# Attention and two mixture layers on one core: the values of dilated pairs are loaded from GpSimd's queue

## The reference

```python
scores = scale * np.matmul(q, k.transpose(0, 1, 3, 2))
rel = pos[:, None] - pos[None, :]
mask_plain = (rel >= 0) & (rel < 32)
mask_dil = (rel >= 0) & (rel < 128) & (rel % 4 == 0)
# heads 0..3 use mask_plain, heads 4..7 mask_dil
attn = softmax(scores under the mask); x = (attn @ v) as rows of 512
# layer 1: each row goes to one of 8 experts (by its cosine to expert_emb), relu(x @ w1[e]) @ w2[e], times a gate
# layer 2: h = x @ w_in; out = (h * cos(h)) @ w_out
```

## Time and profile before

| | us |
|---|---|
| median of 3 runs | 856.87 |
| lowest and highest | 856.0, 858.98 |
| the profiled execution | 854.68 |
| span of its trace | 852.8 |
| TensorE busy | 823.2 (97%) |
| VectorE busy | 608.7 (71%) |
| ScalarE busy | 489.9 (57%) |
| GpSimd busy | 75.7 (9%) |

### The profile page before, as it was taken

The page is one execution under the profiler, slowest core; times in us unless marked ns, Lnnn a source line. Parts: engine busy times, 40 slices in busy tenths (PEclk is TensorE's granted clock), DMA queues, the critical chain, the costliest instruction groups (busy, mean ns, idle before and its releaser), DMA issues.

```text
span 852.8 us, 15550 instructions
## 1 busy us (share of the span) xinstructions
PE 823.2 (97%) x5046; PEld 753.6 (88%) x5046; DVE 608.7 (71%) x1187; ACT 489.9 (57%) x948; POOL 75.7 (9%) x129
## 2 busy tenths in 40 slices
PE   7999999989999999999999999999999999999994
PEld 5778787879999999999989999989999998999993
DVE  7888887876555555555577777798777788777762
ACT  4567767644455454444466666676666676666652
POOL 3112112240100000000000000011000003000002
PEclk9999999999999999999999999999999999999998
DMA  7597886255535434434431211223121214122001
GB/s 148 121 223 180 192 192 197 64 151 170 185 124 162 148 123 125 148 128 144 124 100 52 73 63 62 73 89 111 51 75 50 75 49 149 55 70 67 9 1 74
DMA packets 114913, 93.79 MB, mean 110 GB/s; under 512 B 65816, under 2 KB 94488, under 8 KB 114848
## 3 DMA queue, kind: packets, MB, share of 16 engines
q1 hardware_dynamic: 109920, 78.81, 32.5%
q0 software_dynamic: 4928, 14.16, 5.0%
HBM read 83.51 MB, written 9.44 MB: 109 GB/s over the span
## 4 chain that ended last, share of the span: by engine, by line
PE 84%; DVE 6%; issue 3%; DMA 2%; ACT 2%; POOL 1%; another core or an unknown queue 0%; POOLq 0%; DVEq 0%; ACTq 0%; SPq 0%
PE bank L765 24%; PE bank L763 24%; PE bank L764 24%; PE bank L625 2%; PE bank L604 2%; DMA xtok<-x_rows 2%; PE bank L613 1%; PE bank L588 1%; DVE shifted L1271 1%; DVE row_max L1268 1%; PE bank L706 1%; ACT probs L947 1%; PE bank L805 1%; DMA x_rows<-osb 1%; DVE kT L334 1%
## 5 line engine op out<-in xcount | busy, mean ns | idle before, releaser
L763 PE MATMUL bank<-yh,up_l 128*128 128x384 f32 x384 | 129.4, 337 | 0.5 <-DVE yl L1619 0.5
L765 PE MATMUL bank<-yh,up_h 128*128 128x384 f32 x384 | 129.5, 337 | 0.0
L764 PE MATMUL bank<-yl,up_h 128*128 128x384 f32 x384 | 128.9, 336 | 0.0
L765 PE MATMUL bank<-dn_h,hid 128*128 128x512 f32 x288 | 113.9, 396 | 0.0
L763 PE MATMUL bank<-dn_h,hid 128*128 128x512 f32 x288 | 112.5, 391 | 1.4 <-DVE hid L1597 1.4
L764 PE MATMUL bank<-dn_l,hid 128*128 128x512 f32 x288 | 113.8, 395 | 0.0
L1344 DVE TENSOR_TENSOR dn_l<-dn_raw,dn_h 128x512 fp32r<-128x512 f32 (+1 forms) x79 | 71.8, 909 | 54.5 <-ACT dn_h L998 52.5
L1141 ACT ACTIVATE work<-bank 128x384 f32<-128x384 f32 x96 | 47.2, 492 | 79.7 <-PE bank L765 78.7
L998 ACT ACTIVATE dn_h<-dn_raw 128x512 fp32r<-128x512 f32 (+1 forms) x79 | 63.7, 806 | 41.8 <-PE bank L765 41.8
L1153 ACT ACTIVATE work<-work 128x384 f32<-128x384 f32 x96 | 50.5, 526 | 63.8 <-DVE work L1592 61.8
L763 PE MATMUL bank<-xh,up_l 128*128 128x352 f32 x256 | 83.9, 328 | 2.0 <-DVE XS L1479 1.0
(11 more groups left out here) (212 smaller groups left out, 1692.4 us busy)
## 6 DMA issues: line engine op xcount, KB each, us to landing
up_raw<-in_moe_w_dram SPq DMA_DIRECT2D x32, 512.0 KB, 3.6
dn_raw<-in_moe_w_dram SPq DMA_DIRECT2D x32, 512.0 KB, 3.6
up_raw<-in_moe_w_in_dram SPq DMA_DIRECT2D x24, 512.0 KB, 3.4
dn_raw<-in_moe_w_out_dram SPq DMA_DIRECT2D x24, 512.0 KB, 3.6
qn<-in_q_dram SPq DMA_DIRECT2D x32, 144.0 KB, 2.9
kn<-in_k_dram SPq DMA_DIRECT2D x32, 144.0 KB, 3.3
xtok<-x_rows SPq DMA_DIRECT2D x4, 1152.0 KB, 7.6
x_rows<-osb POOLq DMA_DIRECT2D x8, 288.0 KB, 3.5
```

Source lines behind the costliest of these rows:

```text
L763: mm(o, w[1], x[0], start=first, stop=False, skip_group_check=True)
L764: mm(o, w[0], x[1], start=False, stop=False, skip_group_check=True)
L765: return mm(o, w[0], x[0], start=False, stop=last, skip_group_check=True)
```

## The change

SyncE no longer issues the eight transfers of a dilated pair. GpSimd issues them: behind the store of plain pair p it waits on `pv_done` and loads the values of pair p + 2 of the same batch. They get a semaphore of their own, `dil_v_in`, and TensorE waits on that for pairs 2 and 3. Source, destination and number of the transfers are as before.

```diff
@@ SyncE, load_v and the loop @@
-                    if p < PAIRS // 2:
...
-                    else:
-
-                        vr = vb.rearrange("o (i a r) d -> r i (o a) d", a=2, r=2)
-                        for t, j0, j1, r, i0 in V_PARTS:
-                            sp.dma_start(vw[slot][j0:j1, t:t + 4:3, h, 0:D], vr[r, i0:i0 + j1 - j0]).then_inc(v_in[slot], 16)
...
-                    load_v(b, p)
+                    if p < PAIRS // 2:
+                        load_v(b, p)
@@ GpSimd @@
+            def load_dilated_v(b, p):
+
+                slot = p % 2
+                pool.wait_ge(pv_done, b * STEPS + 3 * p + 3)
+                pool.sem_inc(carrier, 1)
+                for h in range(2):
+                    vr = v[bass.ds(b, 1), 2 * p + h].rearrange("o (i a r) d -> r i (o a) d", a=2, r=2)
+                    for t, j0, j1, r, i0 in V_PARTS:
+                        pool.dma_start(vw[slot][j0:j1, t:t + 4:3, h, 0:D], vr[r, i0:i0 + j1 - j0]).then_inc(dil_v_in[slot], 16)
...
                     if p < PAIRS // 2:
                         pool.dma_start(xb.rearrange("(t p) c -> p t c", p=QT), o).then_inc(stored[slot], 16)
+                        load_dilated_v(b, p + PAIRS // 2)
@@ TensorE, times_v @@
-                    pe.wait_ge(v_in[p % 2], b * (PLAIN_IN + DIL_IN) + (PLAIN_IN if p < 2 else PLAIN_IN + DIL_IN))
+                    pe.wait_ge(v_in[p % 2] if p < 2 else dil_v_in[p % 2], (b + 1) * (PLAIN_IN if p < 2 else DIL_IN))
```

More of the change, by code:

```diff
@@ L199, in fused_kernel @@
         v_in = [sem(f"v_in{i}") for i in range(2)]
+        dil_v_in = [sem(f"dil_v_in{i}") for i in range(2)]
         tr_done = sem_from("tr_done", 8)
@@ L366, in load_v @@
                     vb = v[bass.ds(b, 1), 2 * p + h]
-                    if p < PAIRS // 2:
[L369 to L373, removed]
-                    else:
-                        vr = vb.rearrange("o (i a r) d -> r i (o a) d", a=2, r=2)
-                        for t, j0, j1, r, i0 in V_PARTS:
-                            sp.dma_start(vw[slot][j0:j1, t:t + 4:3, h, 0:D], vr[r, i0:i0 + j1 - j0]).then_inc(v_in[slot], 16)
+                    sp.dma_start(vw[slot][WINDOW:, 0, h, 0:D], vb[:, 0:QT].rearrange("o p d -> (o p) d")).then_inc(v_in[slot], 16)
+                    later_tiles = vb[:, QT - WINDOW:QT - WINDOW + (NT - 1) * QT].rearrange("o (t p) d -> p (o t) d", p=QT)
+                    sp.dma_start(vw[slot][0:QT, 1:NT, h, 0:D], later_tiles).then_inc(v_in[slot], 16)
+                    late = vb[:, QT:NT * QT].rearrange("o (t p) d -> p (o t) d", p=QT)[QT - WINDOW:]
+                    sp.dma_start(vw[slot][QT:P, 1:NT, h, 0:D], late).then_inc(v_in[slot], 16)
             def load_rows(b):
```

## The result

The changed kernel takes 866.13 us (median of 4 runs, 864.78 to 868.03), the kernel before 857.35 (4 runs, 856.0 to 858.98). The ratio is 1.0106, with a 95% interval of 1.0087 to 1.0125: slower by 8.8 us. The profiled execution of the changed kernel is 865.71 us, its span 864.2.

What follows compares the result with a forecast made beforehand. The attention's TensorE-VectorE handover was taken to bound the kernel, so late values count nearly fully. Waits of 0.2 + 0.2 + 0.6 + 2.2 = 3.2 us, added to the 856.87 us median, gave 860.1; range 856.0 to 865.7.

Steps and rivals of the forecast that it cites:

- What bounds the kernel: Attention: TensorE and VectorE hand work over within hundredths of a microsecond, so nearly all of a TensorE wait enters the total.
- Removal, 0: SyncE loses sixteen issues per batch: no gain or loss, row load still landing in 7.4 to 7.9 us.
- a moved wait of ScalarE: Sign of a wrong prediction: ScalarE's wait for the row load, 2.1 us in three, changes.
- Issue, 0: GpSimd's eight loads behind each plain store, 0.67 us apart, fit its idle time and delay no store: 0 us.
- The rival of the dear issue: GpSimd issues a load every 1.28 us instead of 0.67: some 33 us slower, 890; chance 0.04.
- The time left: From the last value load's start on GpSimd to TensorE's need of the values: 2.0 to 3.1 us.
- The landing beside SyncE's transfers: GpSimd's values: 2.6 to 2.9 us among small transfers, 3.3 beside the row load, later beside batch 3's expert weights.
- the second rival: Next batch's queries and keys and the weights lie in the values' way: 8.8 us at worst, 865.7; chance 0.12.
- The terms 0.2 and 0.6: TensorE's waits for pair 2's values in batches 1 and 2, from a landing of 3.3 us: 0.2 and 0.6 us.
- Pair 3 at 0: No TensorE wait for pair 3's values, since waits ahead of pair 2 also put off its need: 0 us.
- The queues hold each other up: SyncE's and GpSimd's queues delay each other more than taken: 8.8 us at worst, 865.7; chance 0.12.
- The values overtake: DMA engines serve queues by turns, every value load lands in 2.6 to 2.9 us: 0.4 us, 857.3; chance 0.27.

Runs made afterwards that it cites:

- e10: Changed kernel, with the next batch's first and second queries and keys held for products, and the first expert weights for the last values; 860.95 us, ratio 1.0042.
- e6: Changed kernel, with GpSimd issuing the dilated pair's value loads ahead of the plain pair's store, not behind it; 862.09 us, ratio 1.0056 to the kernel before.
- e1: Changed kernel, with SyncE holding the next batch's first queries and keys until pair 2's values have landed; 873.05 us, ratio 1.0219 to the kernel before.
- e3: Changed kernel, with the next batch's first queries and keys held until pair 2's values land, and expert weights until the last pair 3's; 872.52 us, ratio 1.0182.
- e8: Changed kernel, with the next batch's first queries and keys held until the products of pair 1 are done; 865.71 us, ratio 1.0092 to the kernel before.
- e12: Changed kernel, with the second head of pair 3's values back on SyncE under its own semaphore; 862.19 us, ratio 1.0057 to the kernel before.
- e2: Changed kernel, with the first expert weights held until pair 3's values of the last batch have landed; 865.37 us, ratio 1.0105 to the kernel before.

## Why the prediction was wrong

**What bounds the kernel: right.** A wait of TensorE ahead of the product went into the total nearly whole, and 8.8 us more are found between the first product and the last.

**Removal, 0: right for the row load's landing, wrong for its wait.** It lands in 7.5 to 7.8 us as in the earlier trace rows. But in batch 3 it is issued late: 0.93 us ahead of the plain store (125.65, 126.58) in place of 2.65, because the store before it stalled, and ScalarE's wait for it holds up TensorE (2.02 us in e10, 2.72 in e6, with no wait for values there). The sum had no term for a stall of GpSimd; nothing in the trace of before shows one. I counted GpSimd's idle time there and its transfers' durations, and that was not enough. The prediction named a moved wait of ScalarE as a sign of being wrong, and it moved, from 2.1 to 4.1 us.

**Issue, 0: right, and a little too dear.** Eight loads take 5.06 to 5.13 us, 0.63 apart and not 0.67, each 0.563 to 0.732 us long, and the next plain store came 7.9 us behind the last (7.8 before). The rival of the dear issue is out: VectorE was busy for 1.55 to 1.92 of every 2 us from 57 to 65, and the longest of the 64 loads took 0.732 us. By the Trainium skill, SBUF — State Buffer, "Who interferes with whom", GpSimd cannot write the descriptors of its transfers while VectorE runs in a two-port mode. The 5.5 us a pair that the prediction put on that did not come about here; whether any operation of VectorE's was of that kind, no run shows.

**The time left: right.** 3.1 us forecast in batch 1, 3.6 measured; in batches 0 and 2 it was 3.0 and 3.6 where 2.4 and 2.7 were forecast. So the prediction did not miss in when the loads are issued but in how long they take to land.

**The landing beside SyncE's transfers: this step failed.** For pair 2 of batches 1 and 2 I took 3.3 us, the best of SyncE's own loads beside the row load, and put the worst at the 5.0 us of the earlier trace rows. It was 5.4 to 7.1, more than either. The earlier trace rows are loads that nothing but the row load stood ahead of; I priced the new ones by them although the order on SyncE had turned around, as the prediction itself says under the second rival. The terms 0.2 and 0.6 were 2.03 + 1.29 and 2.55 us. Batch 0, taken at 0.2 "since the queues are emptier", was 0.95: its loads landed in 2.2 to 3.7 us where 2.6 was taken, and holding queries and keys back there (e1, e3) leaves 0.58 and 0.38 us of a wait of 0.79, so about half of it stays unexplained. For batch 3 I had 2.2 us: the gap is 3.05, of which the wait for values is 1.19 and the rest the late row load, so the size is near and the cause half wrong. Pair 3 at 0 was right only because pair 2 waited, the reason that the prediction gives for it: in e8, where pair 2 of batch 1 no longer waits, pair 3 waits 1.7 us, and the 2.6 to 2.9 us of landing taken for it were 3.6 to 4.6.

**The rivals.** "The queues hold each other up", 8.8 us and 865.7, is what happened, and I gave it 0.12. Its mechanism is shown by e1 (landing 2.3 to 4.3 us without the queries and keys) and e10 (5.8 us back by the pace of SyncE alone). That its sum is the measured difference is partly luck: it had 4.3 us for the values in batch 3, where they cost 1.19, and neither the stall nor the clock. "The values overtake", which I gave 0.27, is out: no landing of pair 2 stayed near 2.9 us beside the row load and the queries and keys. The engines' share was between 0.98 and 1.27 in every window from 57 to 71 us, the last of the queries and keys landed at about 67.2 (58.8 + 8.4), and the last values only 1.2 us behind them, at 68.4. The Trainium skill, DMA: Bandwidth & Descriptors, "Queues, rings and completion order", states that each DMA engine serves its queues in turn, packet by packet. No row here speaks for or against such turns; my reading, which no run shows, is that turns spare nothing when 352 KB in pieces of 256 B need many of them on engines that are already full. The Trainium skill, the same page, "Issuing engines are not separate DMA queues", says that issuing from a second engine saves only the issuing time; e10 and the changed kernel show what it costs besides, namely that the first engine then runs ahead.

**The numbers.** The sum was 3.2 us and the loss 8.8. The range ended at 865.7, where the second rival's worst ends came out, and the time was 0.4 above it. The direction with the largest chance, slower, was right.

## What to carry to other kernels

Before a transfer is taken out of a queue, look at what stood behind it: the issue of the removed transfers was a brake on the next ones, and those may now reach the DMA engines first. Look as well at the transfers that wait for the queue's new owner: here a stall of GpSimd made the row load late, and that cost about as much in batch 3 as the values did. Read the landing time of a load together with the share of the DMA engines in that stretch and with what has been issued just before; a landing time measured in the old order is no price for the new one. And when a gate cures one wait, look at the next transfer in that list before believing it: here three gates were needed (e10), and one or two of them gave back almost nothing or made it worse.

## What the runs showed of the hardware that I had not expected

- GpSimd stalled for 1.4 to 1.7 us between two transfers, after some 15,000 contiguous pieces (in e12 with another 0.51 one transfer on). It is shown in nine kernels and moved in e12; that pieces are what is counted fits two places and is not shown.
- 1.87 us without work were followed by half clock for some 3.4 us in batch 1, a wait of 2.00 us in batch 2 was not. The same came behind 2.29 us in e2, 2.02 in e10 and 2.72 in e6, and not behind 2.05 in e2. What tells them apart was not tried.
- SyncE's two key loads behind the row load took 3.41 us to issue (57.96); those of the next pair at 66.33 took 1.13, and the two in the kernel before 1.01 (61.81). What held the first two up is not shown: the DMA engines' share was 0.98 to 1.27 from 57 to 63 us, and no lower, 1.17, around 66 us.
- The span goes on for 5.9 to 8.8 us behind the last store's issue, and differs by 2.6 us between kernels with the same end. A difference of 0.3% between kernels can come from there, and only the times of the first and last product told it from a gain in the attention.
